# Attention with two experts behind it: weights split once into DRAM scratch, another order of the first sweep, five step buffers, and adds moved to the vector engine

## What is computed

```python
for c in range(24):                       # chunks of 32 queries
    k_full = concat(mem_k, k[l_start:r_end])      # 16 keys to the left, 8 to the right
    a = softmax(q_c @ k_full.T / 8)
    out[c] = a @ concat(mem_v, v[l_start:r_end])
x = out as (3072, 512)
h = x @ moe_w_in                          # 512 -> 1024
solu = h * softmax(h)
x2 = (layernorm(solu) * g_ln) @ moe_w_out # 1024 -> 512
h = x2 @ moe2_w_in                        # 512 -> 2048
g = h * clip(h + 3, 0, 6) / 6
y = g @ moe2_w_out                        # 2048 -> 512
```

## Time and profile before

| | us |
|---|---|
| median of three runs | 1009.35 (1007.37 to 1009.9) |
| the profiled execution's own time | 1009.16 |
| its span, first to last instruction | 1007.4 |
| busy in the span: PE | 928.8 (92%) |
| DVE | 619.0 (61%) |
| ACT | 482.4 (48%) |
| POOL | 440.1 (44%) |
| mean granted TensorE clock | 0.964 |

### The profile page before, as it was taken

How to read it: one execution, slowest core, us unless ns; L and a number is a source line. 1 busy time by engine, 2 the same in 40 slices (tenths; PEclk the granted TensorE clock), 3 DMA queues, 4 the chain that set the end, 5 groups by cost and what they waited for, 6 DMA issues and landing times.

```text
span 1007.4 us, 17791 instructions
## 1 busy us (share of the span) xinstructions
PE 928.8 (92%) x6200; PEld 826.3 (82%) x6200; DVE 619.0 (61%) x904; ACT 482.4 (48%) x1109; POOL 440.1 (44%) x466
## 2 busy tenths in 40 slices
PE   7888999999999998969699999999879899898988
PEld 6767888888888887859478888888678899898987
DVE  3887777777777867636565555554567444635454
ACT  4555565556565655435465554555453342323231
POOL 5352101010112655660623322332449587787963
PEclk8987999999999999989899999999898899999999
DMA  9631233333344686465423333333682333434331
GB/s 192 135 78 36 69 75 74 74 73 73 73 135 127 175 234 198 155 215 196 145 95 135 135 125 134 134 118 115 221 333 63 126 106 125 146 92 137 104 125 63
DMA packets 145694, 130.01 MB, mean 129 GB/s; under 512 B 96504, under 2 KB 108792, under 8 KB 145656
## 3 DMA queue, kind: packets, MB, share of 16 engines
q1 hardware_dynamic: 135896, 99.90, 34.3%
q0 software_dynamic: 5728, 24.12, 7.3%
q10 hardware_dynamic: 4032, 5.51, 1.5%
HBM read 81.01 MB, written 48.50 MB: 129 GB/s over the span
## 4 chain that ended last, share of the span: by engine, by line
PE 32%; POOL 28%; issue 24%; DVE 7%; DMA 4%; ACT 3%; SPq 1%; POOLq 1%; DVEq 0%; ACTq 0%
PE banks L767 18%; POOL gs_raw L677 18%; PE banks L936 3%; POOL ws L565 3%; POOL ws_raw L559 2%; PE banks L721 2%; POOL v_mix L581 2%; PE banks L734 2%; PE banks L690 2%; PE banks L758 2%; PE banks L747 2%; POOL x_mix L605 2%; DMA v_mix_scratch<-v_mix 1%; DVE prob L1223 1%; DMA v_mix<-in_moe_w_out_dram 1%
## 5 line engine op out<-in xcount | busy, mean ns | idle before, releaser
L936 PE MATMUL banks<-vs,gs 128*128 128x256 f32 x2016 | 252.9, 288 | 22.6 <-DVE gs L1199 10.1
L936 PEld LDWEIGHTS banks<-vs,gs 128*128 128x128 f32 x2016 | 249.4, 196 | 26.3 <-issue 12.1
L810 PE MATMUL banks<-xs,ws 128*128 128x512 f32 x1008 | 238.2, 398 | 14.9 <-ACT part L1033 14.8
L677 POOL TENSOR_TENSOR gs_raw<-gs_raw 128x256 f32<-128x256 f32 x192 | 210.3, 1097 | 85.3 <-DMA gs_raw<-g_scratch 73.5
L810 PEld LDWEIGHTS banks<-xs,ws 128*128 128x128 f32 x1008 | 192.4, 192 | 60.0 <-issue 11.5
L1199 DVE TENSOR_TENSOR gs<-gs_raw,gs 128x1792 fp32r<-128x1792 f32 x48 | 106.6, 2237 | 103.6 <-ACT gs L1148 103.6
L1148 ACT CAST gs<-gs_raw 128x1792 fp32r<-128x1792 f32 x48 | 81.2, 1693 | 167.4 <-POOL gs_raw L677 167.4
L767 PE MATMUL banks<-y_t,w_out 128*128 128x384 f32 x768 | 142.4, 341 | 5.7 <-ACT x_out L1006 5.7
L767 PEld LDWEIGHTS banks<-y_t,w_out 128*128 128x128 f32 x768 | 133.9, 190 | 6.5 <-ACT x_out L1006 6.0
L767 PE MATMUL banks<-w_in,x_t 128*128 128x512 f32 x552 | 134.4, 400 | 1.5 <-DVE solu L1253 1.5
L767 PEld LDWEIGHTS banks<-w_in,x_t 128*128 128x128 f32 x552 | 104.0, 192 | 24.1 <-DVE solu L1253 1.4
(11 more groups left out here) (78 smaller groups left out, 1037.4 us busy)
## 6 DMA issues: line engine op xcount, KB each, us to landing
g_scratch<-part SPq DMA_DIRECT2D x96, 256.0 KB, 2.0
gs_raw<-g_scratch SPq DMA_DIRECT2D x48, 512.0 KB, 3.9
v_mix_scratch<-v_mix POOLq DMA_DIRECT2D x8, 896.0 KB, 4.1
vs_raw<-v_mix_scratch SPq DMA_DIRECT2D x8, 896.0 KB, 8.3
q_in<-in_q_dram SPq DMA_DIRECT2D x32, 192.0 KB, 3.8
out_dram<-o_stage SPq DMA_DIRECT2D x12, 512.0 KB, 2.9
k_in<-in_k_dram SPq DMA_DIRECT2D x24, 240.0 KB
v_in<-in_v_dram SPq DMA_DIRECT2D x24, 240.0 KB
```

The costliest lines, as they stand in the source:

```text
L677: nc.gpsimd.tensor_tensor(gs_raw[x][:, to, :], gs_raw[x][:, a, :], gs_raw[x][:, b, :], op).then_inc(gt_done, 1)
L810: mm = pe.matmul(ps, ws[:, a, W_OF[i], kc, :], xs[g][X_OF[i]][:, m, kc, :], start=(fresh and x == 0), stop=(x == len(passes) - 1), skip_gr ...
L936: mm = pe.matmul(m_ps[i][:, s, :], gs[x][:, a, G_OF[i], s * P:(s + 1) * P], vs[p][:, m, V_OF[i], :], start=(p == 0 and s == 0 and n == 0), ...
```

## The change

Five things are changed together.

1. The seven mixes of moe2_w_in, for all eight pairs, and of moe2_w_out for pairs 0 to 3 (`VSPLIT`), are mixed and split into high and low parts by POOL alone and stored to DRAM scratch (`item(n)`, n = 0 to 11); for pairs 4 to 7 of moe2_w_out they are only mixed and stored (n = 12 to 15). `batch(1)` has items 0 to 7, one behind each tile's `normalise`, `batch(2)` items 8 to 15, `batch(3)` the mixes of tokens. All items share one input buffer `raw_mix` and one output buffer. In the first sweep SP loads finished `ws` blocks, 256 KB each, as the block before is used; ACT's `high_ws` and POOL's `mix_ws` and `low_ws` are gone.
2. The first sweep has units (0, 0), (0, 1), (1, 0), (1, 1), (1, 2), ..., (7, 2) and then (8, 0), which is pair 0 with the last 1024 tokens. The last x2 tiles go through DRAM like all others.
3. The second sweep has five `gs` buffers in place of four; its 48 steps are written out and no loop is left in it. `vs` of pairs 0 to 3 needs no split.
4. `mix_gs` moves from POOL to DVE, one step ahead of `low_gs`. In DVE's and ACT's program the end of a group stands behind step 1 of the next one.
5. Places in SBUF and PSUM banks are assigned anew.

The diff, cut to its core (a line of "..." stands for what is left out):

```diff
-        ws = at("ws", 184, [P, 2, 7, 2, P], F32R)
-        ws_raw = at("ws_raw", 198, [P, 7, 2 * P], F32)
-        x_mix = at("x_mix", 184, [P, 7, 2, XT // 2], F32)
-        v_mix = at("v_mix", 198, [P, 7, GH], F32)
+        ws = at("ws", 184, [P, 7, 2, 2, P], F32R)
...
+        raw_mix = at("raw_mix", 198, [P, 7, GH], F32)
+        w_split = at("w_split", 184, [P, 7, 2, GH], F32R)
+        v_split = at("v_split", 184, [P, 2, 7, GH], F32R)
+        NGS = 5
+        G_AT = [0, 14, 28, 184, 80]
+        gs = [at(f"gs{x}", G_AT[x], [P, 2, 7, GH], F32R) for x in range(NGS)]
+        gs_raw = [at(f"gs_raw{x}", G_AT[x] + 7, [P, 7, GH], F32) for x in range(NGS)]
+        V_AT = [42, 56, 136, 150, 94, 108, 122, 168]
...
+        def nth(p, g):
+            return g if type(p) is int and p == 0 else 3 * p + g - 1
+        def unit_before(p, g):
+            if g > 0:
+                return p, g - 1
+            return (0, 1) if type(p) is int and p == 1 else (p - 1, 2)
+        def tokens_of(p, g):
+            return 2 if type(p) is int and p == PAIRS else g
...
+            def load_ws(p, *products):
+                for i in products:
+                    if type(p) is not int or p > 0:
+                        sp.wait_ge(prod_done[i], nth(p, 0))
+                    src = w_dram[p % PAIRS, :, W_OF[i]] if type(p) is int else \
+                        w_dram[bass.ds(p, 1), :, W_OF[i]].rearrange("o p a n -> (o p) a n")
+                    sp.dma_start(ws[:, W_OF[i]].rearrange("p a k n -> p (a k n)").bitcast(F32),
+                                 src.rearrange("p a n -> p (a n)")).then_inc(ws_here[i], 16)
...
+                if p < VSPLIT:
+                    sp.dma_start(vs[p][:, :, :, :].bitcast(F32), v_dram[p]).then_inc(vs_here[p], 16)
+                else:
+                    sp.dma_start(vs_raw[p][:, :, :], vm_dram[p - VSPLIT]).then_inc(vs_here[p], 16)
...
+            unit(PAIRS, 0)
             sp.wait_ge(prod_done[3], 3 * PAIRS)
+            for e in range(6):
+                sp.wait_ge(stored[e], 16 * 14)
+            load_gs(3)
+            load_vs(4)
+            load_gs(4)
+            load_vs(5)
+            load_vs(6)
+            store_g(PAIRS, 0, 12)
             for e in range(6):
                 sp.wait_ge(stored[e], 16 * 2 * PAIRS)
+            load_vs(7)
...
+            for n in range(NGS, NGRP * PAIRS):
+                if n % PAIRS == PAIRS - 1 and n > PAIRS:
+                    for h in (1, 0):
+                        store_out(n // PAIRS - 1, h)
+                sp.wait_ge(*step_used(n - NGS))
+                load_gs(n)
...
+            def load_item(n):
+                if n > PAIRS + VSPLIT:
+                    pool.wait_ge(v_mix_kept, 16 * (n - PAIRS - VSPLIT))
+                elif n > 0:
+                    pool.wait_ge(split_lo, 3 * n)
+                if n < PAIRS:
+                    for j in range(2):
+                        at_col = (n + PAIRS * j) * P
+                        pool.dma_start(raw_mix[:, 2 * j:2 * j + 2, :].rearrange("p s (k n) -> p (s k) n", k=2),
+                                       moe2_w_in.rearrange("(k p) n -> p k n", p=P)[:, :, at_col:at_col + P]
+                                       ).then_inc(w_mix_here, 16)
+                else:
+                    pool.dma_start(raw_mix[:, 0:4, :].rearrange("p (j s) n -> p j (s n)", j=2),
+                                   moe2_w_out.rearrange("(j c p) n -> c p j n", j=2, c=PAIRS)[n - PAIRS]
+                                   ).then_inc(v_mix_here, 16)
+            def mix_item(n):
+                if n < PAIRS:
+                    pool.wait_ge(w_mix_here, 32 * (n + 1))
+                    sums = ((4, 2, 3, ALU.add), (5, 4, 0, ALU.subtract), (6, 1, 5, ALU.subtract),
+                            (2, 0, 2, ALU.subtract))
+                else:
+                    pool.wait_ge(v_mix_here, 16 * (n - PAIRS + 1))
+                    sums = ((4, 1, 0, ALU.subtract), (5, 3, 4, ALU.subtract), (6, 2, 5, ALU.subtract),
+                            (1, 3, 1, ALU.subtract))
+                for x, (to, a, b, op) in enumerate(sums):
+                    if x:
+                        pool.wait_ge(mixed, 4 * n + x)
+                    nc.gpsimd.tensor_tensor(raw_mix[:, to, :], raw_mix[:, a, :], raw_mix[:, b, :], op
+                                            ).then_inc(mixed, 1)
+                pool.wait_ge(mixed, 4 * n + 4)
+                if n >= PAIRS + VSPLIT:
+                    pool.dma_start(vm_dram[n - PAIRS - VSPLIT], raw_mix[:, :, :]).then_inc(v_mix_kept, 16)
+            def split_item(n):
+                if n > 0:
+                    pool.wait_ge(split_kept, 16 * n)
+                for x, (a, b) in enumerate(((0, 2), (2, 4), (4, 7))):
+                    hi, lo = (w_split[:, a:b, half, :] if n < PAIRS else v_split[:, half, a:b, :] for half in (HI, LO))
+                    nc.gpsimd.tensor_copy(hi, raw_mix[:, a:b, :]).then_inc(split_hi, 1)
+                    pool.wait_ge(split_hi, 3 * n + x + 1)
+                    nc.gpsimd.tensor_tensor(lo, raw_mix[:, a:b, :], hi.bitcast(F32), ALU.subtract
+                                            ).then_inc(split_lo, 1)
+                pool.wait_ge(split_lo, 3 * n + 3)
+                if n < PAIRS:
+                    pool.dma_start(w_dram[n], w_split[:, :, :, :].bitcast(F32)).then_inc(split_kept, 16)
+                else:
+                    pool.dma_start(v_dram[n - PAIRS], v_split[:, :, :, :].bitcast(F32)).then_inc(split_kept, 16)
+            def item(n):
+                mix_item(n)
+                if n < PAIRS + VSPLIT:
+                    split_item(n)
+                if n + 1 < 2 * PAIRS:
+                    load_item(n + 1)
...
+                    if items is not None:
+                        item(items + kk)
+                    if tokens and kk in (0, 2, 5):
+                        load_tokens(*{0: (0, 0), 2: (0, 1), 5: (1, 0)}[kk])
+                    if tokens and kk in (1, 3, 6):
+                        mix_tokens(*{1: (0, 0), 3: (0, 1), 6: (1, 0)}[kk])
                     if last and kk == 0:
+                        load_tokens(1, 1)
                     if last and kk == 1:
+                        mix_tokens(1, 1)
...
-            with pool.Fori(1, B - 1) as b:
-                batch(b)
-            batch(B - 1, mix=True)
+            load_item(0)
+            batch(1, items=0)
+            batch(2, items=PAIRS)
+            batch(3, tokens=True)
...
+            unit(0, 0)
+            unit(0, 1)
             for g in range(NX):
+                unit(1, g)
+            with pe.Fori(2, PAIRS) as p:
                 for g in range(NX):
+                    unit(p, g)
+            unit(PAIRS, 0)
+            third(PAIRS, 0)
...
-                    if last and kk == 2:
-                        act.wait_ge(wt_done, 4)
-                        act.wait_ge(ws_free, 1)
-                        high_ws(0, ORDER)
...
+            for n in range(3, NGRP * PAIRS):
+                if VSPLIT <= n < PAIRS:
+                    high_vs(n)
+                high_gs(n)
+                if n % PAIRS == 1:
+                    hold_first(n // PAIRS - 1)
+            hold_first(NGRP - 1)
...
+            def mix_gs(n):
+                x = n % NGS
+                dve.wait_ge(g_here[x], 16 * (n // NGS + 1))
+                for k, (to, a, b, op) in enumerate(((4, 1, 3, ALU.add), (1, 0, 1, ALU.subtract),
+                                                    (5, 4, 0, ALU.subtract), (6, 2, 5, ALU.subtract))):
+                    if k:
+                        dve.wait_ge(gt_done, 4 * n + k)
+                    nc.vector.tensor_tensor(gs_raw[x][:, to, :], gs_raw[x][:, a, :], gs_raw[x][:, b, :], op
+                                            ).then_inc(gt_done, 1)
...
+            unit(0, 0)
+            unit(0, 1, then=[None, None, lambda: low_xs(2, 0), None, None])
+            unit(1, 0, then=[lambda: low_xs(2, 1), None, lambda: low_xs(2, 2), None, None])
+            unit(1, 1, then=[lambda: low_xs(2, 3), lambda: low_xs(2, 4), lambda: low_xs(2, 5), lambda: low_xs(2, 6)])
+            unit(1, 2)
+            with dve.Fori(2, PAIRS - 1) as p:
                 for g in range(NX):
                     unit(p, g)
             last = PAIRS - 1
             unit(last, 0)
             unit(last, 1)
+            unit(last, 2, then=[lambda: mix_gs(0), None, lambda: mix_gs(1)])
+            unit(PAIRS, 0, then=[lambda: low_gs(0), lambda: mix_gs(2), lambda: low_gs(1)])
+            sum_of(PAIRS, 0, 12)
+            gate(PAIRS, 0, 12)
...
+            for n in range(2, NGRP * PAIRS):
+                if VSPLIT <= n < PAIRS:
+                    low_vs(n)
+                if n + 1 < NGRP * PAIRS:
+                    mix_gs(n + 1)
+                low_gs(n)
+                if n % PAIRS == 1:
+                    finish(n // PAIRS - 1)
+            finish(NGRP - 1)
```

(52 more changed lines are left out.)

528 lines of the change are left out of this document (181 added, 347 removed).

## The result

The changed kernel takes 1045.64 us (median of four runs, 1045.41 to 1048.31). The kernel before took 1008.36 us beside it (four runs, 1006.33 to 1009.9). The ratio is 1.0377, with a 95% interval of 1.035 to 1.0404. The span of the profiled execution is 1043.6 us, 36.2 more than before. The direction was forecast. The size was not: 1020 was named. 1045.64 is inside the wide range (975 to 1055) and outside the forecast's own one, 1005 to 1040.

What follows compares the result with a forecast made beforehand. TensorE was taken to bound attention, with losses at the seams. Price 61 us less gains of 7 (first seam), 17 (first sweep) and 26 (second sweep) gives +11 on 1009.2: 1020 us; own range 1005 to 1040, wide range 975 to 1055.

Steps and rivals of the forecast that it cites:

- the price: Batches 1 and 2 of attention: twelve split items on POOL make normalise late and cost 61 us, formula 11 w - 21.
- the first seam: Between attention and first sweep: 7 us gained together, 1.7 from batch 3's dropped mixing and 5 at the seam's waits.
- The wait w: POOL's wait for each raw_mix load queued behind the split store, eleven times; 7.5 us, bounds 3.1 and about 14.
- the rival of the full rate: POOL's queue keeps 0.40 MB per microsecond beside attention's loads: w = 5.6, price 40.5, time 1000 us; chance 0.20.
- POOL's own time: Twelve items in batches 1 and 2: 10.4 us each plus issuing the next loads, 139 us in all.
- the time made up behind the items: After batch 2's late normalise (68 us): 8 us of lateness are free, so TensorE loses 60 us.
- The gain in the first sweep: First sweep takes 233 us in place of 250, a gain of 17; bounds none and 22.
- its ws loads (1.8 MB in 28 us) have three units of time: End of the first sweep: the moved pair 0's weight loads have time enough, with a DMA share of 0.36 there.
- the term for the end of the sweep: End of the first sweep: high_gs and mix_gs stand between ACT's and DVE's copies, 3 us lost.
- The second sweep: Takes 249 us instead of 275.5, a gain of 26 (15 if DVE's chain is late at each boundary, 34 if never).
- POOL's competition goes: Second sweep: argument against the missing-gains rival, as the adds move from POOL to DVE; no size of its own.
- The rival of the missing gains: Slower adds, or the DVE chain late at each second-sweep boundary: 20 of 50 us gains missing, about 1042 us; chance 0.12.

Runs made afterwards that it cites:

- Experiment 1: The changed kernel with each next item's load issued on POOL ahead of the store of the item just split; 1011.32 us, ratio 1.0035 to the kernel before.
- experiment 2: Experiment 1 with items spread six, six and four over batches 1, 2 and 3, none in fourth and eighth tiles of batches 1 and 2; 976.27 us, ratio 0.9672.
- Experiments 4 and 5: First two x loads ahead of ws at the first seam: on the changed kernel 1045.08 us; on experiment 2, with one xs copy a step later, 973.28 us.
- Experiment 3: The changed kernel with the loads of vs 2 and 3 issued behind the last ws block; 1046.06 us, ratio 1.0356 to the kernel before.
- experiment 6: Experiment 2 with vs 2 behind the last ws block, vs 3 behind gs 3, gs 5 and 6 earlier, first-group low_gs(n) ahead of mix_gs(n + 1); 966.27 us.
- Experiments 8 to 10: The changed kernel with the second sweep's adds back on POOL (1052.85 us), with four gs buffers in place of five (1069.64), and with both (1075.71).
- experiment 9: The changed kernel with four gs buffers in place of five, adds still on DVE; 1069.64 us, ratio 1.0628 to the kernel before.

## Why the prediction was right in direction and wrong in size

The changed kernel is 36.2 us longer where +11 was named. The missing 25 us are 8 in the price with the first seam, 14 in the first sweep and 3.5 in the second.

*The price, right in mechanism.* Experiment 1 shows the load behind the store, and experiment 2 shows that the rest of the price is the crowding of the items, with none of it left. The wait w is 7.40 us on average over the eleven loads (7.13 to 8.36), where 7.5 was forecast. The store lands in 7.7 us at the median (moe2_w_in) and 7.1 (moe2_w_out); 7.5 was taken. With that the rival of the full rate (w = 5.6) falls. The figure of the Trainium skill, DMA: Bandwidth & Descriptors, "Anatomy of one DMA", makes an estimated 6.2 us of this store. The trace does not agree: beside attention's loads the measured time is 0.9 to 1.5 us longer.

What was mis-sized is small and lies in three places: POOL's own time, the time made up behind the items, and the seam. POOL's own time for twelve items is 147 us and not 139. The 512-wide copy takes 0.61 us at best and 0.78 on average where 0.52 was drawn from the earlier trace rows; the 512-wide subtraction takes 1.27 against 1.18. The `normalise` of batch 2's fifth tile is 72.1 us late (68 forecast). It would be 75 late, had the first one of batch 1 not started at 102.1 in place of 105.0. That start is spread and not an effect of the change: in the traces of the kernels of this document, whose first batch is the changed kernel's, it lies between 102.1 and 105.9. From there to the start of the seam 6.2 us are made up and not 8.2. At the seam the stretch takes 36.7 us in place of 40.4, a gain of 3.7 where 5 was named. What is late there is what the prediction put there, SP's loads, and they cost 9.3 us of waiting. Experiments 4 and 5 show that the loads alone are not it: with them earlier, DVE's `y_t` or ACT's `x_out` comes last.

*The gain in the first sweep, wrong: 3 us and not 17.* The step that failed is "its ws loads (1.8 MB in 28 us) have three units of time". The time was there, but what SP issues ahead of these loads was not counted, and the term for the end of the sweep stood at 3 us. SP's DMA issues at the end of the sweep, changed kernel:

```profile
761.29 1.69 SPq L390 DMA_DIRECT2D ws<-w_split_scratch  x2
763.03 1.51 SPq L410 DMA_DIRECT2D vs<-v_split_scratch  x3
764.58 1.60 SPq L400 DMA_DIRECT2D g_scratch<-part  x2
766.95 0.34 SPq L390 DMA_DIRECT2D ws<-w_split_scratch  x1
```

The last ws block goes out behind three vs loads and is there 16 us later. These are split weights now, twice as wide as the mixed ones, so they bring 5.5 MB, and the DMA engines are 97% busy from 750. TensorE waits:

```profile
783.24 2.90 PE L835 MATMUL banks<-xs,ws 128*128 128x512 f32 x6 [8.30 <-DMA ws<-w_split_scratch]
```

Of the 12.6 us by which 540.4 to 785.9 is longer than the 233 forecast, this stretch holds the greater part. Its 35.9 us have 94 matmuls, 21 us at 0.225, so 15 are lost where 3 were counted. The last 1.3 of the 14 us are ahead of 540. The middle is as forecast: 664 matmuls in 150 us are 0.226 each. Experiment 3 gives back 9 us of the stretch by moving two of those loads, and experiment 6 gives back 10 and keeps them.

*The second sweep, right in size (22.5 of 26), wrong in cause.* The first group loses 11.3 us (54.7 less 366 matmuls at 0.1185) where 10 were counted. PE waits for `gs` of step 4 behind `mix_gs(5)`, which stands for the load of step 5, as the prediction had it; the load came 22.8 us into the group and not 18.5. The boundaries after it cost nothing, also as named. The add takes 0.424 us (0.42 forecast), the subtraction 2.02. The other 2 to 3 us are matmuls of 0.120 us in place of 0.1185 in the long stretch (1650 of them, 2.9 us). But the prediction put the gain down to POOL leaving the second sweep ("POOL's competition goes") and gave the fifth buffer half a sentence. Experiments 8 to 10 turn this round: 21 us are the buffer's and 4 the adds', and the rest of the change took some of it back. The rows of before allowed for that: four adds of 1.10 us are 4.4 us, less than the 5.0 of a step, so POOL's slow adds were covered as long as a step's data was there in time.

The rival of the missing gains had named about 1042, which is nearer to the measured time than the forecast. That is luck: its mechanism was DVE late at each boundary of the second sweep, and there the boundaries cost nothing. Of the 43 us of gains in the two sweeps 17 are missing, 14 of them in the first sweep, where it had put none.

## What to carry to other kernels

Here a load waited for what was issued ahead of it on its DMA queue (7.4 us behind a store of 1.84 MB, 2.5 to 4.9 ahead of it). So a load whose buffer is free goes ahead of a large store, and a small load that TensorE needs next ahead of large ones for later; here the one exchange was worth 34 us and the other, with its companions, 10. Work on a helper engine costs little by its sum and much by its place: POOL's items delayed the first sweep by 62 us where each stood in the way of the next `normalise`, and not at all with their loads early, six in a batch and the tiles without a `normalise` left free. Where two changes meet in one stage, take each away alone before you name the cause of the gain.

## What the runs showed of the hardware that was not expected

- In the second sweep of experiment 9 a pause of TensorE costs half as much again. Behind each of its five pauses of 2.1 to 2.7 us about 3 us pass at a granted clock of 0.50 to 0.62 (0.50 is 1.2 GHz), in which 14 to 17 matmuls run where 26 would at 0.1185 us. In the changed kernel a pause of 1.88 us at 835 is followed by a clock of 1.00, and the one of 5.09 us at 807 by 3.5 us at 0.52 with 16 matmuls.
- POOL's 128x512 copy takes 0.61 us at best and 0.91 in the item of experiment 1 above, and its 128x256 add 0.76 us on average in attention against 1.15 in the second sweep, where DVE's subtractions grow from 2.02 to 2.33 us. Moving the adds to DVE was worth some 4 us of a second sweep of 253.
